# Banded attention before two mixture-of-experts layers on one core: half-height query loads, a three-operation mask, first loads in order of use, a looped general path on TensorE

## What is computed

```python
scores = scale * np.matmul(q, k.transpose(0, 1, 3, 2))
rel = pos[:, None] - pos[None, :]
is_global = pos[None, :] < int(n_global)              # n_global = 8
is_local = (rel >= 0) & (rel < int(n_local))          # n_local = 96
keep = is_global | is_local
dist = np.where(is_global & ~is_local, float(n_local), np.abs(rel))
scores = np.where(keep, scores - slopes * dist, -1e9)
a = softmax(scores)
out = np.matmul(a, v)
```

## Time and profile before

| | |
|---|---|
| median of 3 executions | 793.82 us (793.75 to 794.51) |
| the profiled execution | 794.11 us |
| its span, first to last instruction | 792.4 us |
| PE, DVE, ACT busy share of the span | 94%, 69%, 58% |
| first product on PE | 14.33 us |
| last product of the attention stage on PE | near 220 us |
| moved by DMA | 151.65 MB |

### The profile page before, as it was taken

The page is one execution under the profiler, slowest core; times in us unless marked ns, Lnnn a source line. Parts: engine busy times, 40 slices in busy tenths (PEclk is TensorE's granted clock), DMA queues, the critical chain, the costliest instruction groups (busy, mean ns, idle before and its releaser), DMA issues. The chain is left out here.

```text
span 792.4 us, 15792 instructions
## 1 busy us (share of the span) xinstructions
PE 740.9 (94%) x5585; PEld 662.7 (84%) x5588; DVE 548.1 (69%) x1499; ACT 461.7 (58%) x931; POOL 165.9 (21%) x189
## 2 busy tenths in 40 slices
PE   2899999999959999999999839999999999999997
PEld 2799999999938888898888627888888888889895
DVE  6878778777477979887777667767675758585420
ACT  3889899899535555565545315454636363636360
POOL 8100000000030232222321202142323232323221
PEclk9999999999969999999999959999999999999999
DMA  8999988986264676545763126676767676759751
GB/s 178 218 212 247 242 213 232 203 233 155 98 211 156 223 248 229 188 143 196 252 232 113 36 77 210 187 222 186 222 185 220 186 223 186 221 169 314 230 120 43
DMA packets 64106, 151.65 MB, mean 191 GB/s; under 512 B 12294, under 2 KB 15750, under 8 KB 64016
## 3 DMA queue, kind: packets, MB, share of 16 engines
q1 hardware_dynamic: 52512, 114.77, 49.2%
q0 software_dynamic: 11504, 35.72, 18.0%
HBM read 118.84 MB, written 16.67 MB: 171 GB/s over the span
## 5 line engine op out<-in xcount | busy, mean ns | idle before, releaser
L2006 PE MATMUL r_ph<-r_xh,r_w1h 128*128 128x384 f32 x256 | 90.7, 354 | 0.0
L2006 PE MATMUL r_ph<-r_xh,r_w1l 128*128 128x384 f32 x256 | 86.2, 337 | 0.0
L2006 PE MATMUL r_ph<-r_xl,r_w1h 128*128 128x384 f32 x256 | 85.8, 335 | 0.0
L604 ACT ACTIVATE pr<-pr,nmx 128x232 f32<-128x232 f32 (+1 forms) x192 | 79.9, 466 | 4.3 <-DVE nmx L710 2.9
L710 DVE CUSTOM_DVE_ANT_0 pr<-sc,bias 128x232 f32<-128x232 f32 (+1 forms) x192 | 65.0, 375 | 19.0 <-PE sc L478 17.7
L611 ACT ACTIVATE prt<-tp 128x384 f32<-128x384 f32 (+1 forms) x128 | 65.4, 536 | 20.4 <-PE tp L490 16.9
L2020 PE MATMUL r_py<-r_w2h,r_hh 128*128 128x512 f32 x192 | 76.3, 398 | 0.0
L2020 PE MATMUL r_py<-r_w2h,r_hl 128*128 128x512 f32 x192 | 75.1, 391 | 0.0
L2020 PE MATMUL r_py<-r_w2l,r_hh 128*128 128x512 f32 x192 | 74.9, 390 | 0.0
L518 PE MATMUL op<-vo,prt 128*128 128x128 f32 x384 | 69.5, 276 | 3.7 <-ACT prt L611 1.9
L477 PE MATMUL sc<-kk,qh 128*128 128x256 f32 x192 | 59.0, 328 | 14.7 <-POOL alive L439 14.3
(11 more groups left out here) (340 smaller groups left out, 1970.4 us busy)
## 6 DMA issues: line engine op xcount, KB each, us to landing
r_w<-moe_w SPq DMA_DIRECT2D x64, 512.0 KB, 5.7
m_w<-moe_w SPq DMA_DIRECT2D x36, 512.0 KB, 6.3
row_buf<-moe_w SPq DMA_DIRECT2D x9, 2048.0 KB, 8.4
r_w2l<-r_w POOLq DMA_DIRECT2D x32, 512.0 KB, 5.4
k_raw<-kI SPq DMA_DIRECT2D x64, 208.0 KB, 6.8
q_raw<-qT SPq DMA_DIRECT2D x64, 192.0 KB, 7.3
vo<-vL SPq DMA_DIRECT2D x16, 384.0 KB
x_rows<-row_buf SPq DMA_DIRECT2D x4, 1536.0 KB, 6.2
```

What stands on the lines that cost most here:

```text
L604: nc.scalar.activation(pr[n % PRS][:, t, lo:CW], pr[n % PRS][:, t, lo:CW], ACT.Exp, bias=nmx[n % PRS][:, t:t + 1], scale=-1.0).then_inc(ex ...
L2006: last = nc.tensor.matmul(ph[m % 4][:, 0:CAP], w[:, c, m * P:(m + 1) * P], x[:, c, :], start=(c == 0 and a == 0), stop=(c == KC - 1 and a ...
```

## The change

- Raw q is loaded once, into partitions 0 to 63: three transfers a head instead of four. The q tile `qq` holds q-high (ACT, 64 partitions) above q-low (DVE, written to partitions 64 to 127). k-high is a full 128-row copy `kh`; k-low is `kl`, used in partitions 0 to 63 alone. The first product has 128 rows, the second 64. The zeros of `ql` are no longer written; the count `FILLS` goes from 24 to 23.
- The mask is made in three full-width operations (`outside`, `far`, `dist`), in units of 2^-40 so that a value outside the mask is huge by itself. It needs `rel_units` (one operation before the wait for `ints`) and `local_units` (one of one column). `pen` is gone; `biases` are plain tensor_scalar operations. POOL adds an affine_select over 256 columns before `RELS`, which goes from 9 to 10.
- `dist` and the biases of head 0 come after the low parts of head 0; the low k of head 1 comes after the first maxima. Biases of the other heads are made at n%3 = 2, one head before use. In steps 0 to 5 the splits of pair 1 come one step later.
- The limits are loaded by ACT's queue; SP's first transfers are k and q of heads 0 and 1, then V of pair 0, then pair 1.
- In the general path, PE's twelve written-out turns become a body of two (two heads) inside one more loop; the order of turns is changed on all engines, and SP loads one query tile at a time there.

```diff
@@ scores (PE) @@
-                        nc.tensor.matmul(to, qh[s][:, hh, q], kk[s][:, hh, keys], start=True, stop=False)
-                        last = nc.tensor.matmul(to, ql[s][:, hh, q], kk[s][:, hh, keys], start=False, stop=True)
+                        nc.tensor.matmul(to, qq[s][:, hh, q], kh[s][:, hh, keys], start=True, stop=False)
+                        last = nc.tensor.matmul(to, qq[s][0:D, hh, q], kl[s][0:D, hh, keys], start=False, stop=True)
@@ loads (SP) @@
                     for half in range(2):
-                        w = slice(half * D, half * D + D)
-                        sp.dma_start(k_raw[s][w, hh, :], kI[g, hh]).then_inc(raw_loaded[s][hh], 16)
-                        sp.dma_start(q_raw[s][w, hh, :], qT[g, hh * D:hh * D + D]).then_inc(raw_loaded[s][hh], 16)
+                        sp.dma_start(k_raw[s][half * D:half * D + D, hh, :], kI[g, hh]).then_inc(raw_loaded[s][hh], 16)
+                    sp.dma_start(q_raw[s][0:D, hh, :], qT[g, hh * D:hh * D + D]).then_inc(raw_loaded[s][hh], 16)
...
-                sp.dma_start(ints[:, 0:1], n_global.partition_broadcast(P)).then_inc(ints_loaded, 16)
-                sp.dma_start(ints[:, 1:2], n_local.partition_broadcast(P)).then_inc(ints_loaded, 16)
                 load_raw(0)
-                load_head(1, 0)
                 load_v(0)
-                load_head(1, 1)
+                load_raw(1)
                 load_v(1)
@@ general path (PE) @@
-                        general_turns(pe, b, turn)
+                        with pe.Fori(0, H // 2) as j:
+                            with pe.Fori(0, QT_N) as i:
+                                at(pe, d_loaded, (H // 2) * PAIR_LOADS * b + PAIR_LOADS * j + 16 * i + 48)
+                                for hh in range(2):
+                                    turn(TURNS * b + 2 * QT_N * j + 2 * i + hh, hh)
@@ split (ACT) @@
-                    dst, src = (kk[s][:, hh, :], k_raw[s][:, hh, :]) if is_k else (qh[s][:, hh, :], q_raw[s][:, hh, :])
+                    dst, src = (kh[s][:, hh, :], k_raw[s][:, hh, :]) if is_k else (qq[s][0:D, hh, :], q_raw[s][0:D, hh, :])
@@ start (ACT) @@
+                act.dma_start(ints[:, 0:1], n_global.partition_broadcast(P)).then_inc(ints_loaded, 16)
+                act.dma_start(ints[:, 1:2], n_local.partition_broadcast(P)).then_inc(ints_loaded, 16)
@@ split (ACT), placing @@
-                        g, c = n // 6 + 1, n % 6 - 1
+                        g, c = n // 6 + 1, n % 6 - (2 if n < 6 else 1)
@@ biases (DVE) @@
-                        v.scalar_tensor_tensor(out=dst[:, h, :], in0=dist[:, w], scalar=-slope, in1=pen[:, w],
-                                               op0=ALU.mult, op1=ALU.add).then_inc(biased, 1)
+                        v.tensor_scalar(dst[:, h, :], dist[:, w], -slope / UNIT, None, ALU.mult).then_inc(biased, 1)
@@ fast (DVE) @@
-                    mask(link, rel[:], kpos[:], lims, isg[:], loc[:], tmp[:], dist[:], between=first_parts)
-                    link(v.tensor_scalar(pen[:], tmp[:], 1.0, BIG, ALU.subtract, ALU.mult))
+                    link(v.tensor_scalar(local_units[:], lims[:, 1:2], UNIT, None, ALU.mult))
+                    link(v.tensor_scalar(outside[:], kpos[:], lims[:, 0:1], None, ALU.is_ge))
+                    link(v.scalar_tensor_tensor(out=far[:], in0=rel[:], scalar=lims[:, 1:2], in1=rel_units[:], op0=ALU.is_ge, op1=ALU.max))
+                    for c in (0, 1):
+                        split(0, c)
+                    link(v.scalar_tensor_tensor(out=dist[:], in0=outside[:], scalar=local_units[:], in1=far[:], op0=ALU.max, op1=ALU.min))
                     biases(0)
-                    dve.wait_ge(biased, 3)
-                    split(0, 2)
                     for n in range(STEPS):
                         if n < ALL_UNITS:
                             maxima(n)
-                        if n == 0:
-                            split(0, 3)
-                        if 1 <= n < H:
-                            biases(n)
+                        if n < 2:
+                            split(0, 2 + n)
+                        if n % 3 == 2 and n // 3 + 1 < H:
+                            biases(n // 3 + 1)
```

More of the change, by code:

```diff
@@ L92, in search_tables, with mask @@
     return flips, steps
-def mask(link, rel, kpos, lims, isg, loc, keep, dist, shift=0.0, between=None):
+def mask(link, rel, kpos, lims, isg, loc, keep, dist, shift=0.0):
     v = link.eng
@@ L221, in build @@
             ints = tb("ints", [P, 2], I32)
-            rel, kpos, isg, loc, tmp, dist, pen = (tb(x, [P, CW + P]) for x in ("rel", "kpos", "isg", "loc", "tmp", "dist", "pen"))
+            rel, kpos, rel_units, far, outside, dist = (tb(x, [P, CW + P]) for x in ("rel", "kpos", "rel_units", "far", "outside", "dist"))
+            fits, local_units = tb("fits", [P, 1]), tb("local_units", [P, 1])
             bias, bias0 = tb("bias", [P, H, CW]), tb("bias0", [P, H, P])
@@ L245, in fb @@
                 return banded_only.enter_context(nc.sbuf_tensor(name, shape, dt))
-            qh = [fb(f"qh{s}", [P, 2, S], F32R) for s in range(2)]
-            ql = [fb(f"ql{s}", [P, 2, S], F32R) for s in range(2)]
-            kk = [fb(f"kk{s}", [P, 2, KW], F32R) for s in range(2)]
+            qq = [fb(f"qq{s}", [P, 2, S], F32R) for s in range(2)]
+            kh = [fb(f"kh{s}", [P, 2, KW], F32R) for s in range(2)]
+            kl = [fb(f"kl{s}", [P, 2, KW], F32R) for s in range(2)]
             banded_only.close()
@@ L313, in general_turns @@
                 with eng.Fori(0, H // 2) as j:
-                    for hh in range(2):
-                        for i in range(QT_N):
-                            body(TURNS * b + 2 * QT_N * j + QT_N * hh + i, j, hh, i)
+                    for i in range(QT_N):
+                        for hh in range(2):
+                            body(TURNS * b + 2 * QT_N * j + 2 * i + hh, j, hh, i)
             block = st.enter_context(nc.Block())
@@ L554, in fast, with turn @@
                             gate_products(q)
-                def turn(g, j, hh, i):
+                def turn(g, hh):
                     r = hh * D
-                    if i == 0 and hh == 0:
-                        at(pe, d_loaded, 4 * g + 48)
                     at(pe, d_maxed, g)
                     for c in range(2):
-                        last = nc.tensor.matmul(sp_[c][:, 0:S // 2], qd[r:r + D, i * P:(i + 1) * P],
+                        last = nc.tensor.matmul(sp_[c][:, 0:S // 2], qd[r:r + D, 0:P],
                                                 kd[r:r + D, c * (S // 2):(c + 1) * (S // 2)], start=True, stop=True)
@@ L754, in fast @@
                                 norm(nlink, hd)
-                        g, c = n // 6 + 1, n % 6 - 2
+                        g, c = n // 6 + 1, n % 6 - (3 if n < 6 else 2)
                         if g < PAIRS and 0 <= c < PARTS:
                             split(g, c)
+                        elif n == 6:
+                            split(1, PARTS - 1)
                         for b in range(B):
@@ L762, in fast, with turn @@
                     open_route(link)
-                def turn(b, h, i):
+                def turn(g, h, i):
                     LINKS = 6
-                    g = TURNS * b + QT_N * h + i
                     link = Chain(dve, d_chain, LINKS * g)
@@ L805, in general @@
                         settle(dve, passed)
-                        with dve.Fori(0, H) as h:
+                        with dve.Fori(0, H // 2) as j:
                             with dve.Fori(0, QT_N) as i:
-                                turn(b, h, i)
+                                with dve.Fori(0, 2) as hh:
+                                    turn(TURNS * b + 2 * QT_N * j + 2 * i + hh, 2 * j + hh, i)
                         gate_dve(dve, b, logits, lp, G1, gsems)
```

36 lines of the change are left out of this document (18 added, 18 removed).

## The result

The changed kernel takes 866.46 us (median of 4, 862.43 to 875.61) against 793.79 for the kernel before on the same chip, 72.7 us slower. The ratio, 1.090 with a 95% interval of 1.086 to 1.0935, leaves out the 875.61, a run in the chip's slower state. The forecast was 789.3 and faster. The profiled execution took 862.43 us, its span is 860.7, 68.3 more than before.

What follows compares the result with a forecast made beforehand. PE was taken to bound attention from 37 us, its late first product the start. First product -3.1, first maxima -0.4, ramp -1.0 sum to -4.5 us: 789.6 profiled, 789.3 median; range 786.8 to 797.

Steps and rivals of the forecast that it cites:

- the second score product with 64 rows: Attention units on PE: cutting this product's rows costs nothing, as L521 with 104 rows; taken at 0 us.
- full switch price: Rival, attention on PE: each 64-row product left and re-entered at 0.19 us, 192 times, 36.5 us, giving 825.8; chance 0.19.
- my far end: Second score product: the other end kept beside 0, 0.19 us out and back, from L1960's 8-column products.
- PE's branch: Before the first product: PE's jump over the general path stalls on a fetch; shortened, the stall goes, PE ready near 7.5 us.
- the packet on queue 8: Sign before the first product: a 0.02 MB instruction packet, read as PE's branch target being fetched; expected to be gone.
- the loop does nothing: Rival, attention start: branch still misses or the 2.7 us had another cause; -0.5 to -2 us, 791.8 to 793.3; chance 0.10.
- The flag: Kernel start: limits, sharing DMA engines with k and q data, land 0.4 us later than 4.88, between 0 and 1.0.
- First maxima: DVE's L710 after the first scores: from 16.03 to 12.5 us, -3.5, so 0.4 us more gained.
- The ramp: Attention up to 37 us: fewer DVE bias pairs and lighter loads starve PE less; -1.0 us, ends -3 and +0.5.
- The long part: Attention from 37 to 200 us: PE busy 162.63 of 163 us and never waiting, so earlier gains are kept.
- Behind attention: Expert layers after attention: untouched by the change, about 570 us of the span only move along.
- Raw loads at nothing: Long part of attention: 32 raw q transfers fewer gain nothing, as that part is PE-bound.

Runs made afterwards that it cites:

- Experiment 3: Experiment 1's kernel with the second score product cut from 128 to rows 0 to 95: 790.54 us, ratio 0.9958 to the kernel before.
- experiment 1: Changed kernel with the second score product on 128 rows again, GpSimd filling the lower half of `kl` with zeros: 791.18 us, ratio 0.9953 to the kernel before.
- experiment 2: Kernel before with only its second score product cut to 64 rows: 864.84 us, ratio 1.0879.
- experiment 4: Changed kernel with both 128-row score products first, then both 64-row ones, two changes a unit instead of four: 822.16 us, ratio 1.035 to the kernel before.
- experiment 5: Changed kernel with the 64-row product on 128 of its 256 key columns: 857.11 us, ratio 1.0771 to the kernel before.
- after: The changed kernel itself, with the whole change, beside the kernel before: 866.46 us, ratio 1.090.
- experiment 6: Changed kernel with k-low written to all 128 partitions and a 128-row second product, no zeros: 790.15 us, ratio 0.9952 to the kernel before.
- experiment 7: Experiment 1's kernel with PE's twelve general turns written out again instead of looped: 793.72 us, ratio 0.9992 to the kernel before.
- experiment 11: Experiment 10's kernel with GpSimd's `lane_grid` fill moved behind its wait for the table loads: 788.41 us, ratio 0.9933 to the kernel before.
- experiment 9: Experiment 6's kernel with raw q loaded into both halves of the raw tile again: 790.72 us, ratio 0.9958 to the kernel before.
- experiment 10: Experiment 6's kernel with the two limits loaded first on SP's queue again: 790.22 us, ratio 0.9947 to the kernel before.
- experiment 8: Kernel before with only PE's general path put in loops of one body: 795.67 us, ratio 1.0022.

## Why the prediction was wrong

**The step that failed** is the term "the second score product with 64 rows", taken at 0. I had two rows: L521 with 104 rows, free, and L1960 with 8 columns, 0.19 us for out and back. I took the first as the nearer because it cuts rows too. Experiment 3 shows what it hid: 96 rows, like the 104 of L521, cost what 128 cost, so L521 never was a case of a change. Experiments 1 and 2 put the whole loss on this edit from both sides. Experiments 4 and 5 give the price: about 0.18 us for each change between products of 128 and of 64 rows, with 256 columns or 128. At unit 95, after and experiment 6 differ by 273.0 - 202.2 = 70.8 us, over 384 changes 0.18; 10.9 of them are there at unit 12, some 2 us more than 48 such changes, for the full clock came 9.3 us later. The rival "full switch price" was right in kind, but its price was for out and back, so the sum came to 36.5 us. The kernel pays 0.37 for out and back. Even my far end was half of the truth: L1960 changes the columns of the weights, 8 for 128, and keeps its 128 rows, so it was no row for this change either. That rival was what the Trainium skill says (TensorEngine Tiling (Array Packing), Key Properties): a change of tiling mode, not of the tile alone, drains TensorE. The trace agrees: no weight load runs ahead across a change (0.32 us from load to load instead of 0.12), and 96 and 104 rows are on the free side. I gave that rival a chance of 0.19; with a rule that names this very change, and a row that by the same page stays in the full mode and so can't speak against it, it should have been the likeliest case.

**No slack to hide in.** I had noted that PE has none from 37 us on. That was right: the switches took 70.8 us of PE's time up to unit 95, and none of it was hidden.

**The start, without that step.** Experiment 6 is the change without the switches. Its gain is 4.4 us by the medians and 3.8 by the ratio, where I had 4.5 for the rest. That this fits is in part luck, since the parts came out differently.
- *PE's branch*: the stall was real and the loop takes it away. 7.34 us became 0.37, and experiment 7 brings it back for 2.5 us. But the sign that I read it from, the packet on queue 8, is in every kernel, with the stall and without; only the length of the branch tells them apart. The rival "the loop does nothing" is out for the stall. It would have followed from the 2,048 resident instructions that the Trainium skill gives for PE (Runtime: NRT & Kernel Launch, Instruction fetch mechanics); the 7.34 and 8.44 us speak against that figure.
- *The flag*: limits at 5.77 to 5.96, not 4.88 + 0.4. The delay is 0.9 to 1.1, at the bound of 1.0 that I kept for the range. First product 11.70 to 11.87, not 11.2.
- *First maxima*: 13.13, not 12.5; in after 14.18, because four cold products of 0.51 us stand ahead.
- *The ramp*: about right. Experiment 6 is 2.9 us ahead at the first maxima and 4.2 at unit 12, so 1.3 us are gained between, where I took 1.0.
- *The long part* I took as full. From unit 12 to unit 95 experiment 6 gains another 1.3 us. By the starts of the products 0.9 of them lie between the last score product of a unit and its first transpose, so small waits did stand there before. No run shows which part of the change took them away.
- *Behind attention* I expected a mere shift. The span from the start of unit 95 on is 584.7 us before, 586.0 in experiment 6 and 585.8 in 11, 587.7 in after and 587.8 in 1. So 1 to 3 us are given back there. The half-clock stretch at the hand-over (13.7 us before, 10.2 in 6, 13.7 in 11, 17.1 in 1 and after) does not order these numbers: experiment 7 has 17.1 too, and 585.1 us. PE's waits for gathered rows in the second expert layer go with them (PE's waits before, then in experiment 6):

```profile
PE r_ph L1992 <- DMA r_xg<-x_rows,rows: 0.9, 1, 0.9
```

```profile
PE r_ph L1994 <- DMA r_xg<-x_rows,rows: 2.4, 3, 0.9
```

  They are 0.9 us before and in experiment 2, 1.0 in 7, 1.7 in after, 2.4 to 2.5 in 6 and 11, 3.0 in 1. In after, 1.5 us more pass from the start of unit 95 to the first wide product of the first expert layer, 0.7 of them by the four changes of unit 95 itself. Why the gathers come late stays open.
- *Raw loads at nothing* in the long part: the times of experiment 9 don't speak against it, and by its one trace the lighter loads are worth 0.8 us at unit 95.

## What to carry to other kernels

Cutting a product of TensorE to fewer rows saved nothing in any run here, and with 64 rows it cost about 0.18 us at every change to and from full height. Fill the other rows with something harmless, keep 96 rows or more, or at least put the short products together, which halves the price for two of them. And where a row of the trace is to stand for a new case, ask first whether it is on the same side of the limit: 104 rows beside 128 said nothing about 64. Last, a sign that is to prove a cause, like the packet on queue 8, should be looked for in a kernel without the effect too.

## What the runs showed that was not expected

- One GpSimd operation can hold up DVE, depending on the form of DVE's operation. A tensor_scalar pair of 0.41 us took 3.00 beside `lane_grid`'s fill and 1.38 when it met its last part; `rel_units` took 1.71 instead of 0.43 beside a memset. The scalar_tensor_tensor pairs of the kernel before stayed at 0.59 beside the same fill (kernel before, POOL and DVE):

```profile
18.82 3.32 POOL L447 IOTA lane_grid<- 128x3072 bf16 x1
```

```profile
19.22 0.59 DVE L694 SCALAR_TENSOR_TENSOR bias<-dist,pen 128x128 f32<-128x128 f32 x2
...
21.43 0.59 DVE L694 SCALAR_TENSOR_TENSOR bias<-dist,pen 128x128 f32<-128x128 f32 x2
```

  So the mask in three operations made the biases cheaper and at the same time open to this. The Trainium skill (SBUF — State Buffer, SBUF: two separate sides) has the rule: an operation of DVE that uses both its ports for one operand and one of GpSimd exclude each other for the whole instruction, while one with two inputs is blocked only by a GpSimd operation that reads. Experiments 10 and 11 agree with it: the tensor_scalar pair waited for a fill that only writes, and the two-input pairs did not.
- A branch of TensorE over written-out code cost 7.34, 7.60 and 8.44 us (before, experiments 2 and 7) at a time when loads kept the DMA engines full. Taking it away alone gained nothing (experiment 8).
- The full clock came later in the kernels with changes of height at the start. With four of them a unit it was granted 17.4 us after the first product in after (at 29.3 us), 21.9 in experiment 2 and 41.5 in experiment 5; with two a unit (experiment 4) after 11.6, with none after 2.9 to 10.6 in the nine others, 8.3 in experiment 6. The spread among kernels that do nearly the same is large (2.9 in experiment 9), so single values say little. The same holds for pauses: in experiment 8 one of 1.96 us was followed by 3.4 us at half clock, in the kernel before one of 1.88 us at the same place was not.
